# Transposed activations in a fused decayed attention, mixture of experts and cosine MLP: all attention first, then half-width feed-forward loops over all tokens

## The reference

```python
# attention, blocks of 64 positions, decay lam per head
intra = einsum('bhic,bhjc->bhij', qb, kb) * Dmask[None]      # Dmask = lam^(i-j), i >= j
out[:, :, sl] = einsum('bhij,bhjd->bhid', intra, vb) + einsum('bhid,bhde->bhie', qb * lam_pow, kv_state)
kv_state = lam_block * kv_state + einsum('bhsd,bhse->bhde', kb * rev_pow, vb)
# 4 experts, D 512, F 1024
p = domain_probs / (domain_probs.sum(-1, keepdims=True) + 1e-09)
out += p[:, e:e + 1] * (np.maximum(x @ w1[e], 0.0) @ w2[e])
# MLP, D 512, F 2048
h = x @ w_in
return (h * np.cos(h)) @ w_out
```

## Time and profile before

| | |
|---|---|
| median of 3 runs | 866.95 us (866.77 to 867.06) |
| span of the profiled execution | 864.7 us |
| PE busy | 844.6 us (98%), 4080 instructions |
| PEld busy | 699.8 us (81%) |
| DVE busy | 381.4 us (44%) |
| ACT busy | 211.7 us (24%) |
| POOL busy | 100.7 us (12%) |
| DMA | 41.24 MB, mean 48 GB/s |

### The profile page before, as it was taken

How to read it: one execution, slowest core, us unless ns; L and a number is a source line. 1 busy time by engine, 2 the same in 40 slices (tenths; PEclk the granted TensorE clock), 3 DMA queues, 4 the chain that set the end, 5 groups by cost and what they waited for, 6 DMA issues and landing times.

```text
span 864.7 us, 10883 instructions
## 1 busy us (share of the span) xinstructions
PE 844.6 (98%) x4080; PEld 699.8 (81%) x4080; DVE 381.4 (44%) x560; ACT 211.7 (24%) x362; POOL 100.7 (12%) x78
## 2 busy tenths in 40 slices
PE   6899999999999999999999999999999999999998
PEld 5787887888888888888888888888788888788886
DVE  6725416324130334120234131334949295939393
ACT  2320100123110122110122120232615143615151
POOL 3202102000000000000000000000304141313131
PEclk9999999999999999999999999999999999999999
DMA  7702303132100031100031100031020003210101
GB/s 246 231 13 81 113 0 109 38 97 61 37 0 0 0 97 53 44 0 0 0 97 49 49 1 1 0 97 25 12 61 1 0 0 98 49 49 0 49 0 49
DMA packets 19320, 41.24 MB, mean 48 GB/s; under 512 B 2400, under 2 KB 2400, under 8 KB 19296
## 3 DMA queue, kind: packets, MB, share of 16 engines
q1 hardware_dynamic: 19296, 40.93, 15.3%
HBM read 37.78 MB, written 3.15 MB: 47 GB/s over the span
## 4 chain that ended last, share of the span: by engine, by line
PE 80%; issue 12%; DVE 4%; DMA 2%; POOL 1%; SPq 0%; ACT 0%; POOLq 0%; DVEq 0%
PE ps L642 40%; PE ps L623 38%; DMA slots<-att_in 2%; DVE slots L508 1%; POOL qdec L232 1%; DVE kdec L375 1%; POOL state L243 1%; PE ps L558 1%; PE ps L610 1%; DVE slots L518 1%; DVE slots L503 1%; PE ps L569 0%; DVE w_lo L409 0%; DVE state L395 0%; DVE y L534 0%
## 5 line engine op out<-in xcount | busy, mean ns | idle before, releaser
L623 PE MATMUL ps<-x_hi,w_hi 128*128 (+1 forms) x576 | 225.5, 391 | 2.4 <-DVE slots L518 1.4
L642 PE MATMUL ps<-w_hi,h_hi 128*128 128x512 f32 x576 | 224.1, 389 | 1.2 <-issue 1.2
L623 PE MATMUL ps<-x_hi,w_lo 128*128 (+1 forms) x576 | 224.2, 389 | 0.0
L623 PE MATMUL ps<-x_lo,w_hi 128*128 (+1 forms) x576 | 224.2, 389 | 0.0
L642 PE MATMUL ps<-w_lo,h_hi 128*128 128x512 f32 x576 | 224.1, 389 | 0.0
L642 PE MATMUL ps<-w_hi,h_lo 128*128 128x512 f32 x576 | 224.1, 389 | 0.0
L273 ACT ACTIVATE h_hi<-ps 128x512 fp32r<-128x512 f32 x96 | 57.5, 599 | 364.1 <-PE ps L623 364.1
L428 DVE SCALAR_TENSOR_TENSOR h_lo<-ps,h_hi 128x512 fp32r<-128x512 f32 x96 | 66.4, 692 | 177.7 <-ACT h_hi L273 177.7
L250 POOL TENSOR_TENSOR h_lo<-slots,h_hi 128x512 fp32r<-128x512 f32 x48 | 71.0, 1485 | 625.7 <-ACT h_hi L326 625.7
L623 PEld LDWEIGHTS ps<-x_hi,w_hi 128*128 128x128 f32 x576 | 108.1, 188 | 27.5 <-DVE slots L518 3.2
L642 PEld LDWEIGHTS ps<-w_hi,h_hi 128*128 128x128 f32 x576 | 108.1, 188 | 23.9 <-issue 1.6
(11 more groups left out here) (44 smaller groups left out, 357.7 us busy)
## 6 DMA issues: line engine op xcount, KB each, us to landing
w_raw<-w_in SPq DMA_DIRECT2D x96, 256.0 KB, 2.8
slots<-att_in SPq DMA_DIRECT2D x24, 512.0 KB, 4.6
out<-y SPq DMA_DIRECT2D x12, 256.0 KB, 2.1
dp<-dp_in SPq DMA_DIRECT2D x1, 24.0 KB, 4.7
lam<-lam_in SPq DMA_DIRECT2D x1, 6.0 KB, 1.7
```

What stands on the lines that cost most here:

```text
L623: mm = pe.matmul(ps[:, f % H_BANKS, :], w[:, 0, f, at], x[:, k, xs], start=(k == 0 and n == 0), stop=(k == KT - 1 and n == 2))
L642: mm = pe.matmul(ps[:, Y_BANK + t, :], h[:, f, at], w[:, 1, f, :], start=(f == 0 and n == 0), stop=(f == FT - 1 and n == 2))
```

## The change

All 12 attention units run first, in pairs (one unit of each batch element), with four slots for the loads, three PSUM banks for the results and one for both increments. A unit's tokens go to their place in natural order, so a chunk is 512 successive tokens.

Then come 12 halves of 512 hidden units over all tokens. A half has 12 up groups (order f, then chunk c) and 12 down groups (order c, then 128 output features d), each of 12 matmuls into one of eight banks. In the down product the weights are stationary and h moves, so y is transposed like x, and TensorE's transposes and `y_tr` are gone. The probabilities of an expert are normalised as 12x128 rows, written to a scratch tensor in HBM and loaded back broadcast to all partitions (`prob(e)`, 768 KB each); VectorE scales relu(h) by them (h >= 0 times p) into a ring `r_ring`, ACT copies the high part and POOL subtracts for `h_lo`. y is added up in SBUF; after half 7, ACT and POOL split it into x. The output is stored transposed. h_hi and h_lo hold a whole half. Weight pieces are loaded and split at fixed groups (`piece_order`). All loops are written out.

```diff
+    within = [(3, 0, 1, 0), (4, 1, 0, 2), (5, 1, 0, 3), (6, 0, 1, 1), (9, 0, 1, 2),
+              (12, 0, 1, 3), (15, 1, 1, 0), (18, 1, 1, 1)]      # (group, kind, halves ahead, f)
...
+            for h in range(HALVES):                              # gpsimd
+                for f in range(HF):
+                    for c in range(CHUNKS):
+                        i = UP * h + CHUNKS * f + c
+                        pool.wait_ge(s_hhi, i + 1)
+                        r = r_ring[:, i % R_RING, :] if h < MLP else gg[:, i % 2, :]
+                        pool.tensor_tensor(h_lo[:, f, chunk(c)], r, f32(h_hi[:, f, chunk(c)]),
+                                           ALU.subtract).then_inc(s_hlo, 1)
...
+            for p in range(BLOCKS):                              # vector, attention
+                mask(2 * p)
+                mask(2 * p + 1)
+                if p + 1 < BLOCKS:
+                    if p + 2 < BLOCKS:
+                        k_decay(2 * p + 2)
+                        k_decay(2 * p + 3)
+                    update(p)
+                piece(p)
+                x_low(2 * p)
+                x_low(2 * p + 1)
+                if p == 0:
+                    normalise()
...
+            for h in range(MLP, HALVES):                         # vector, MLP
+                for i in range(UP + 1):
...                                        # L503, L508, L512 of unit i, then L518 of unit i - 1
+                    if i < UP:
+                        pieces_after(h, i)
+                for i in range(UP, GROUPS):
+                    pieces_after(h, i)
+                    down(h, i)
...
+            for p in range(BLOCKS):                              # tensor, attention
+                if p:
+                    from_state(2 * p)
+                    from_state(2 * p + 1)
+                if p + 1 < BLOCKS:
+                    increment(2 * p)
+                    increment(2 * p + 1)
+                from_scores(2 * p)
+                from_scores(2 * p + 1)
+                if p + 1 < BLOCKS:
+                    scores(2 * p + 2)
+                    scores(2 * p + 3)
...
+            def down(h, c, d):
+                g = down_group(h, c, d)
+                if c == 0 and d == 0:
+                    pe.wait_ge(s_wlo, PLACE[1, h, HF - 1] + 1)
+                if d == 0:
+                    pe.wait_ge(s_hlo, UP * h + CHUNKS * (HF - 1) + c + 1)
+                pe.wait_ge(s_free, g - BANKS + 1)
+                for f in range(HF):
+                    s = (HF * h + f) % W2_SLOTS
+                    at = slice(P * d, P * (d + 1))
+                    for n, (w, x) in enumerate(((w2_hi, h_hi), (w2_hi, h_lo), (w2_lo, h_hi))):
+                        mm = pe.matmul(ps[:, g % BANKS, :], w[:, s, at], x[:, f, chunk(c)],
+                                       start=(f == 0 and n == 0), stop=(f == HF - 1 and n == 2))
+                mm.then_inc(s_mm, 1)
+
+            for h in range(HALVES):
+                for f in range(HF):
+                    for c in range(CHUNKS):
+                        up(h, f, c)
+                for c in range(CHUNKS):
+                    for d in range(KT):
+                        down(h, c, d)
```

More of the change, by code:

```diff
@@ L33 @@
 KT = D // P
+TOKENS = BATCH * SEQ
+BLOCKS = SEQ // P
+UNITS = BATCH * BLOCKS
+EXPERTS, PARTS = 4, 6
 FT = 8
[L35 to L42, removed]
+HF = FT // 2
+HALVES = 2 * PARTS
+CT = 512
+CHUNKS = TOKENS // CT
+GROUPS = HF * CHUNKS + KT * CHUNKS
+UP = HF * CHUNKS
+BANKS = 8
 RING = 4
-FIRST_TR = EXPERTS * CHUNKS - 2
+W2_SLOTS = 6
+R_RING = 4
+SLOTS = 4
+MLP = 2 * EXPERTS
 INV_2PI = 0.15915494309189535
@@ L53, with piece_order, up_group, down_group @@
 R_MIN = -4.7123885
[L56 to L64, removed]
+def piece_order():
+    at_start = [(0, 0, 0), (0, 0, 1), (0, 0, 2), (0, 0, 3), (1, 0, 0), (1, 0, 1)]
+    within = [(3, 0, 1, 0), (4, 1, 0, 2), (5, 1, 0, 3), (6, 0, 1, 1), (9, 0, 1, 2),
+              (12, 0, 1, 3), (15, 1, 1, 0), (18, 1, 1, 1)]
+    order, after = list(at_start), {}
+    for h in range(HALVES):
+        for i, kind, ahead, f in within:
+            if h + ahead < HALVES:
+                after[h, i] = len(order)
+                order.append((kind, h + ahead, f))
+    return order, after, len(at_start)
+ORDER, AFTER, AT_START = piece_order()
+PLACE = {piece: q for q, piece in enumerate(ORDER)}
+def up_group(h, f, c):
+    return GROUPS * h + CHUNKS * f + c
+def down_group(h, c, d):
+    return GROUPS * h + UP + KT * c + d
+def build(nc, att_in, lam_in, dp_in, w_in, p_scr, out):
     ctx = ExitStack()
@@ L155, in _ @@
         def _(sp):
[L156 to L169, removed]
@@ L205, in _ @@
[L205 to L215, removed]
@@ L270, in moe_chunk @@
[L270 to L280, removed]
-                    for k in range(FT):
-                        piece(e + 1, k)
@@ new lines, in x_high, with pieces_after @@
+            def x_high(n):
+                act.wait_ge(s_intra, n + 1)
+                act.activation(x_hi[:, :, columns(n)],
+                               ps[:, X_BANK + n % X_BANKS, :].rearrange("p (a n) -> p a n", a=PAIRS),
+                               ACT.Copy).then_inc(s_xhi, 1)
+            def pieces_after(h, i):
+                if (h, i) in AFTER:
+                    piece(AFTER[h, i])
+            for p in range(BLOCKS):
+                piece(p)
+                x_high(2 * p)
+                x_high(2 * p + 1)
@@ new lines, in update, with x_low @@
+                    up = ps[own, INC_BANK, :].rearrange("p (b a n) -> p b a n", b=BATCH, a=PAIRS)
+                    if p == 0:
+                        ins = dve.tensor_copy(st, up)
+                    else:
+                        ins = dve.tensor_tensor(st, up, st, ALU.add)
+                ins.then_inc(s_st, 1)
+            def x_low(n):
+                dve.wait_ge(s_xhi, n + 1)
+                dve.tensor_tensor(x_lo[:, :, columns(n)],
+                                  ps[:, X_BANK + n % X_BANKS, :].rearrange("p (a n) -> p a n", a=PAIRS),
+                                  f32(x_hi[:, :, columns(n)]), ALU.subtract).then_inc(s_xlo, 1)
@@ new lines, in _, with down @@
+            k_decay(0)
+            k_decay(1)
+            for p in range(BLOCKS):
[6 more added lines that the diff above has]
+                    update(p)
+                piece(p)
+                x_low(2 * p)
+                x_low(2 * p + 1)
+                if p == 0:
+                    normalise()
+            def down(h, i):
+                c, d = (i - UP) // KT, (i - UP) % KT
+                g = GROUPS * h + i
+                dve.wait_ge(s_mm, g + 1)
+                at = y[:, d, chunk(c)]
+                if h in (0, MLP):
+                    if h == MLP:
+                        dve.wait_ge(s_x2lo, KT * c + d + 1)
+                    dve.tensor_copy(at, ps[:, g % BANKS, :]).then_inc(s_free, 1)
+                else:
+                    dve.tensor_tensor(at, ps[:, g % BANKS, :], at, ALU.add).then_inc(s_free, 1)
@@ new lines, in _ @@
+            for h in range(MLP):
+                e = h // 2
+                dve.wait_ge(s_p[e], 16)
+                for i in range(UP):
+                    g, n = GROUPS * h + i, UP * h + i
+                    dve.wait_ge(s_mm, g + 1)
+                    if n >= R_RING:
+                        dve.wait_ge(s_hlo, n - R_RING + 1)
+                    dve.scalar_tensor_tensor(out=r_ring[:, n % R_RING, :], in0=ps[:, g % BANKS, :], scalar=0.0,
+                                             in1=prob(e)[:, chunk(i % CHUNKS)], op0=ALU.max,
+                                             op1=ALU.mult).then_inc(s_free, 1)
+                    pieces_after(h, i)
+                for i in range(UP, GROUPS):
+                    pieces_after(h, i)
+                    down(h, i)
@@ new lines, in increment @@
+            def increment(n):
+                pe.wait_ge(s_kd, n + 1)
+                for a in range(PAIRS):
+                    for par in range(2):
+                        own = slice(DH * par, DH * (par + 1))
+                        of = slice(DH * (2 * a + par), DH * (2 * a + par + 1))
+                        at = D // 2 * (n % 2) + DH * a
+                        mm = pe.matmul(ps[own, INC_BANK, at:at + DH], kdec[:, n % 2, of], slots[:, n % SLOTS, 3, of],
+                                       start=(n % 2 == 0 and a == 0), stop=(n % 2 == 1 and a == PAIRS - 1),
+                                       skip_group_check=True)
+                mm.then_inc(s_inc, 1)
@@ L659, in _ @@
-            with pe.Fori(0, CHUNKS) as c:
-                chunk(PARTS - 1, c, last_mlp=True)
+            scores(0)
+            scores(1)
+            for p in range(BLOCKS):
+                if p:
[9 more added lines that the diff above has]
+                    scores(2 * p + 3)
@@ new lines, in up @@
+            def up(h, f, c):
+                g = up_group(h, f, c)
+                if c == 0:
+                    pe.wait_ge(s_wlo, PLACE[0, h, f] + 1)
```

(12 more changed lines are left out.)

601 lines of the change are left out of this document (235 added, 366 removed).

## The result

The changed kernel takes 897.23 us (median of 4 runs, 895.13 to 898.58), the kernel before beside it 867.0 us (866.77 to 867.9): 1.035 times as long, 95% interval 1.0331 to 1.0369. The forecast was 898, and the profile shows that nearly every term of its sum was where it was said to be. One, the attention, was right only as a sum, its parts missing in opposite directions.

What follows compares the result with a forecast made beforehand. TensorE's matmuls were taken as the floor, 783.4 us. With attention 57, new waits 41.0, slow matmuls 10.8 and tail 3.5 the span was 895.7, plus 2.2 around it 897.9 us; range 880 to 908.

Steps and rivals of the forecast that it cites:

- the attention: All attention units ahead of the first up matmul: 57 us against 67.3 before, with bounds of 52 and 63.
- Matmuls: Up and down loops: still 3456 matmuls of the same shape and pace, so the term stays 783.4 us.
- Transposes, splits, old waits: In the MLP: transposes gone, -5.2 us; old MLP waits gone, -5.0; splits of y and scaled Relu cost 0.
- rival (d): Expert phase stalls too, say by prob or piece loads; 0.5 us a half would give 902; chance 0.04.
- Pair 1: Second pair of attention units, with the normalisation ahead of its masks: 10.3 us.
- Pairs 2 to 4: Middle attention pairs, at 8.3 us a pair of VectorE work with hops: 24.9 us.
- the landing of a load: kv loads in the attention: released 6.3 us before they are needed, taking 4.6 us to land.
- Rival (c): Loads bound the attention, 14.9 MB at 252 GB/s: attention 65 us, in all 906; chance 0.09.
- The pauses: TensorE waits for h_lo of unit 9: 10.5 us in halves 8, 9 and 10, 9.5 in half 11, sum 41.0.
- One sign that I had named: VectorE's clamp L512 in the MLP units: 1.40 us expected in the profile after; 0.43 would speak for (b).
- rival (b): POOL and VectorE don't collide in MLP units: four pauses of some 4 us, no slow matmuls, 862; chance 0.09.
- The slow matmuls: Matmuls behind each of the four new pauses lose 2.7 us, 10.8 in all, with bounds of 0 and 13.

Runs made afterwards that it cites:

- The first experiment: Changed kernel with the up groups of halves 8 to 11 run chunk by chunk instead of f by f: 847.7 us, 0.977 of the kernel before.
- The second experiment: Changed kernel with POOL's h_lo subtraction in halves 8 to 11 covering 32 of 512 columns: 860.33 us, 0.9925 of the kernel before.
- the fill: Changed kernel with 44 extra matmuls ahead of the wait for h_lo in each of halves 8 to 11: 890.22 us, 1.027 of the kernel before.
- the kernel with both repairs: Changed kernel with up groups of halves 8 to 11 chunk by chunk and the normalisation ahead of the first k_decay: 842.37 us, 0.9717 of the kernel before.

## Why the prediction was right, point by point

*Matmuls.* 783.4 stood: 32.64 us per 144 in every undisturbed phase, with weights or with activations as the stationary operand.

*Transposes, splits, old waits.* Their 10.2 us went, and what was costed at nothing cost nothing. Halves 0 to 7 run without a gap, 522.5 us from 58.28 to 580.82 against 522.2, so rival (d) falls.

*Attention.* 57 forecast, 58.3 measured, but two terms were wrong and partly cancelled, which was luck. The start was right (17.5; the first from_state began at 17.34). Pair 1 was put at 10.3 and took 14.6: I had given the normalisation some 2 us, and it took 5.4, because its small two-input additions waited for POOL; that is 3.4 of the 4.3, and the wait it caused brought the slow `from_scores` of 3.68 us with it, which the forecast didn't have. Pairs 2 to 4 were put at 24.9 and took 22.5: VectorE did its 8.3 a pair once (masks at 31.38 and 39.67; the next pair took 9.2), but TensorE had fallen behind in pair 1 and caught up, and the narrow increments took 0.5 us a unit, not the 1.0 that I kept. Two sizes were off badly. One is the 2 us for the normalisation, whose collision could have taught. The other is the landing of a load, put at 4.6 us: the page of after gives 7.4 at the median, and the chain holds one of 6.94 (from 36.88), which made the pair at 39.67 one of 9.2 us. Rival (c) as priced falls, since the attention took 58.3 and not 65; but the loads are not free of the path: VectorE waited 0.6 us for one in the changed kernel's pair 3 and 1.6 in that pair with the normalisation out of the way.

*The pauses.* 41.0 forecast, 41.1 measured: 10.5, 10.6, 10.6 and 9.5 against three of 10.5 and one of 9.5. The h_lo of unit 9 was due at 43.1 and came at 43.0. The first experiment shows that the order is the cause; the second shows that most of its length comes from POOL: 2.6 instead of 10.5, of which 1.1 is the cut of the subtraction itself, as worked out ahead, and the rest the collision.

By the rule of the Trainium skill cited there (SBUF — State Buffer, "Who interferes with whom") the trace agrees in after as well; the same section adds that two SBUF inputs are enough for VectorE to collide, which the 1.25 us of a 12x128 addition shows.

One sign that I had named was misread: the clamp's median is 0.43 after and not 1.40. In units with a piece the collision hits the second range step instead (1.38); the sum of a unit, 3.67, stays. Whoever had taken the clamp's median alone would have called rival (b) right.

*Tail and rest.* 3.5 forecast, 3.4 measured; the 2.2 us around the span were 1.85.

*The slow matmuls.* 10.8 forecast, 10.1 measured, and the fill took 9.1 of them away at waits that were all but unchanged. Here my bound from the start of the run, 2.7 us after 6.3 us of idle time, held roughly for all pauses of 4.5 to 10.6 us in the profiles (1.6 to 3.2). That a pause of 2.6 us can cost the same, and that waits of 0.81 and 1.42 us can cost some 1.4, was outside what the earlier trace rows suggested, where 1.71 us cost nothing.

The Trainium skill, TensorE: Matmul & The Clock Gate, "The HAM clock gate", has this drop to 1.2 GHz; after the change the clock column shows it (0.69 and 0.81), so the trace agrees. At the start of the run the column said 1.00 over matmuls of twice their length, and there the matmuls' durations decide.

*Rival (b)* gave 862 for a world without the collision. The second experiment built most of that world, with a subtraction that is itself 1.1 us shorter, and gave 860.3.

## What to carry to other kernels

When a loop is widened so that the second product needs the results of all its first groups at once, don't count how busy the engines are; count at which moment the first dependent group wants its last input, and put the groups in the order in which the consumer takes them. Here the same instructions cost 49.5 us more in one order than in the other. A pause of TensorE costs more than its length: 1.6 to 3.2 us of slow matmuls came behind each of the twelve pauses of 4.5 to 10.6 us in the MLP of the three profiles that have them. And where a product waits, look for small VectorE instructions ahead of it that run beside POOL: the normalisation took 5.4 us beside POOL and 2.7 without it.

## What the runs showed of the hardware that I had not expected

- In one profile TensorE pauses of 2.3 to 2.7 us were followed by matmuls at the lower clock in two of four cases (1.9 and 3.2 us lost) and not in the others (0.3); the totals of two faster runs of the same kernel leave no room for such a loss. Pauses of 5.5 us cost as much as those of 10.5 us each time.
- A stretch with 8 matmuls between waits of 0.81 and 1.42 us was followed by the lower clock too (0.50, in the kernel with both repairs).
- A VectorE addition of 12 partitions by 128 columns took 0.3 us alone and 1.25 us beside a GpSimd multiplication of 128x512: how small it is doesn't protect it.
